# Retention slot reordered on TensorE, and the last output products and stores with it

## The chip, the cores and the metric

The kernel runs on one core of a Trainium2 chip. The metric is the device time in microseconds. Five engines work side by side and meet at semaphores: TensorE (PE, matmuls), VectorE (DVE), ScalarE (ACT), GpSimd (POOL) and SyncE (SP), which here only issues DMA transfers. An engine takes its instructions strictly in the order of the program, so an instruction that waits holds up everything behind it on its engine. Before the change the kernel took 467.58 us (median of 3 runs, 467.53 to 468.03).

## The reference

Three stages, for 2 sequences of 768 tokens and 512 channels (8 heads of 64):

```python
# 1. retention, per head
for t in range(S):
    state = gamma * state + outer(k[:, :, t], v[:, :, t])
    y[:, :, t] = scale * einsum('bhd,bhde->bhe', q[:, :, t], state)
# 2. low-rank mix over the tokens, then a channel MLP
h = xt @ U @ V                    # xt: tokens last; rank 32
u = x + h.transpose(0, 2, 1)
x = u + relu(u @ w_ch1) @ w_ch2   # 512 -> 2048 -> 512
# 3. spatial gating
h = relu(x @ w_in); u, v = halves of h
v_n = normalised v
gated = u * (w_spatial @ v_n + b_spatial)
out = gated @ w_out               # 512 -> 512
```

## The kernel before, in words

**Retention.** The work is cut into 8 items (`NI`), each a pair of heads of one batch entry; items 0 to 3 are the first sequence. An item has 6 chunks of 128 tokens (`NC`), in two groups g = 0, 1 of three (`G`). For item i TensorE runs:

- `scores(i, g)`: k times q inside a chunk, for both heads, into banks 0 and 1 (`sc_ps`). 64 rows of the array by 128 columns. VectorE (`mask_a`) and ACT (`sc_copy`) take them out, and GpSimd (`mask_b`) applies the second mask.
- `kv(i, c0, c1)`: key-value products of chunks c0 to c1, each 64x64 per head, into bank 4 and, for the fifth, into the unused end of another bank (`kv_out`). They read the keys that ACT has weighted in `decay_k(i)`, which needs the decay table `tab`. VectorE makes the five running states from them (`states`), one after the other.
- `outputs(i, g)`: for each chunk the state before it times q (line 1499), and then the masked scores times v (line 1505), into banks 2 and 3 (`y_ps`). The last chunk reads the fifth state. ACT copies them out (`xt_copy`).
- `turn(i, g)`: six transposes of the outputs, which ACT (`xn_copy`) and VectorE (`xn_rest`) split into a rounded part and its remainder.
- `down(i)`: times U, and `up(i)`: times V. `up` writes 768 columns into two banks, and VectorE adds them to the item's output (`u_add`), which makes `u`.

The token mixing of an item runs in the slot of the next: iteration i of the loop at line 1550 has the scores of i, the transposes of i-1, the products and outputs of i, and `down` and `up` of i-1. All buffers are double (`k = i % 2`). SyncE loads q and k of item i+2 when the scores of item i are done, its table and values when the outputs of item i are done.

**The rest.** The channel MLP runs in 24 steps (`product`, `ch2`), then come the input projection and the spatial product. All large products are split in a rounded part and a remainder, three matmuls for one, and seven block products replace eight (`ORDER` is the order in which the seven are taken; `S_OF` and `T_OF` name sums of weight or token blocks that ACT rounds and VectorE takes the remainder of). The last seven (`out_product`) make the output of the second sequence. Three of its four blocks are sums of two results (`sum_oc`), stored by `store_block`; the fourth is copied by ACT and stored in two halves of 192 KB.

Of the kernel before, what the change touches and what calls it, by code (L numbers as in the profile page):

```python
# [5 lines left out]
def retention_mlp_spatial_gating_kernel(  # L6
# [40 lines left out]
    with ctx:  # L47
# [263 lines left out]
        NN = NT * NP  # L311

# [100 lines left out]
        ORDER = (0, 3, 2, 1, 4, 5, 6)  # L413
        ORDER_B = (0, 3, 2, 1, 4, 5, 6)
# [5 lines left out]
        def _(sp):  # L420
# [83 lines left out]
            sp.wait_ge(stored, 16 * (CT + 1))  # L504
# [92 lines left out]
        def _(act):  # L597
# [284 lines left out]
            def last_copy(m):  # L882
                if m == 0:
                    for c in range(2, CT):
                        act.wait_ge(stage_free[c], 16)
                act.wait_ge(op_done, 7 + m)
                nc.scalar.activation(stage[:, 2 + m, 0:HS], xo_ps[m][:, 0:HS], ACT.Copy).then_inc(last_sb, 1)
# [74 lines left out]
            round_os(2)  # L962
            round_ob(4)
            round_ob(5)
            copy_op(1)
            copy_op(2)
            round_os(3)
# [6 lines left out]
        def _(dve):  # L974
            nc.vector.memset(raw(hh[0])[:, 0, :], 0.0).then_inc(idle_zeroed, 1)
            nc.vector.memset(kv_ps[:, :], 0.0).then_inc(zeroed, 1)
            nc.vector.memset(kv_out(NC - 2), 0.0).then_inc(zeroed, 1)
# [12 lines left out]
            def states(i, c0, c1):  # L990
                k = i % 2
                dve.wait_ge(kv_done, 2 * i + (2 if c0 else 1))
                for c in range(c0, c1):
                    if c:
                        dve.wait_ge(state_done, (NC - 1) * i + c)
                    if c == 0:
                        m = nc.vector.tensor_copy(st[k][:, 0, :], kv_out(0))
                    else:
                        m = nc.vector.scalar_tensor_tensor(
                            out=st[k][:, c, :], in0=st[k][:, c - 1, :], scalar=tab[k][:, 4 * P:4 * P + 1],  # L1000
                            in1=kv_out(c), op0=ALU.mult, op1=ALU.add)
# [27 lines left out]
            def u_add(i):  # L1029
                for h in range(2):  # L1030
                    dve.wait_ge(h_done, 2 * i + h + 1)
                    s = batch_of(i) * S + h * HS
                    nc.vector.tensor_tensor(u[:, pair_of(i), s:s + HS], (h_ps, p_ps)[h][:, 0:HS],
                                            xT[i % 2][:, h * HS:(h + 1) * HS], ALU.add).then_inc(u_done, 1)
# [111 lines left out]
            dve.wait_ge(zeroed, 2)  # L1146
# [4 lines left out]
            for i in range(1, NI):  # L1151
                mask_a(i, 0)
# [21 lines left out]
                u_add(i - 1)  # L1174
            xn_rest(NI - 1, 0)

            for t in range(NT):
                for j in range(NP):
# [42 lines left out]
                    if n == 1:  # L1221
                        u_add(NI - 1)
# [105 lines left out]
            def rest_os(s):  # L1328
                dve.wait_ge(os_hi, s + 1)
# [17 lines left out]
            def rest_ob(q):  # L1347
                dve.wait_ge(ob_hi, ORDER_B.index(q) + 1)
# [10 lines left out]
            def sum_oc(n):  # L1359
                ps, p, i, j = ((zo_ps, po1, 0, 0), (xo_ps, po5, 1, 1), (yo_ps, po16, 0, 1))[n]  # L1360
                dve.wait_ge(op_done, 4 + n)
                dve.wait_ge(op_copied, (1, 2, 3)[n])
                for c in range(2 * i, 2 * i + 2):
                    dve.wait_ge(stage_free[c], 16)
                for m in range(2):
                    k = nc.vector.tensor_tensor(stage[:, 2 * i + m, j * HS:(j + 1) * HS], ps[m][:, 0:HS], p[:, m, :],
                                                ALU.add)
                k.then_inc(oc_sum, 1)
# [61 lines left out]
            rest_ob(1)  # L1430
            rest_os(2)
            rest_ob(4)
            rest_ob(5)
            rest_os(3)
# [7 lines left out]
        def _(pe):  # L1442
# [21 lines left out]
            def kv(i, c0, c1):  # L1464
                k, r = i % 2, i // 2
                if c0 == 0:
# [3 lines left out]
                    else:  # L1470
                        pe.wait_ge(k_decayed, i + 1)
                        pe.wait_ge(v_loaded[k], 16 * r + 16)
                        pe.wait_ge(state_done, (NC - 1) * i)
                for c in range(c0, c1):
# [3 lines left out]
                    for a in range(2):  # L1478
                        h = slice(a * DH, (a + 1) * DH)
                        m = mm(kv_out(c)[h, h], kd[k][:, c, h], att[k][:, 3, c * P + a * DH:c * P + (a + 1) * DH],  # L1480
# [3 lines left out]
            def outputs(i, g):  # L1484
# [11 lines left out]
                for c in range(first, (g + 1) * G):  # L1496
                    for a in range(2):
# [12 lines left out]
            def turn(i, g):  # L1510
                pe.wait_ge(xt_done, 2 * i + g + 1)
                pe.wait_ge(eye_loaded, 16)
                if g and i:
                    pe.wait_ge(u_done, 2 * i - 1)
# [5 lines left out]
            def down(i):  # L1520
                pe.wait_ge(xn_lo, 2 * i + 2)
                pe.wait_ge(ust_lo, 1)
                if i == NI - 1:
                    pe.wait_ge(u_done, 2 * i)
# [4 lines left out]
            def up(i):  # L1529
                pe.wait_ge(p_lo, i + 1)  # L1530
                pe.wait_ge(v_lo, 1)
                for h in range(2):
                    mm((h_ps, p_ps)[h][:, 0:HS], pst[:, :], vst[:, h * HS:(h + 1) * HS],
# [7 lines left out]
            keep_busy(2)  # L1541
            scores(0, 0)
            keep_busy(2)
            pe.wait_ge(zeroed, 2)
# [5 lines left out]
            for i in range(1, NI):  # L1550
                scores(i, 0)
                turn(i - 1, 0)
                turn(i - 1, 1)
                if i == 1:
                    scores(i, 1)
                kv(i, 0, NC - 2)
                kv(i, NC - 2, NC - 1)
                if i > 1:
                    scores(i, 1)
                down(i - 1)  # L1560
                outputs(i, 0)
                outputs(i, 1)
                up(i - 1)
# [36 lines left out]
            def ch2(n, g):  # L1600
                h, c = g // CT, g % CT
                k, j = n % 2, n % NP
                if c == 0:
# [3 lines left out]
                    else:  # L1607
                        pe.wait_ge(w2_lo, 2 * n + h - 1)
                if j == 0 and n and h == 0:
# [49 lines left out]
            product(0, 0)  # L1659
            product(0, 1)  # L1660
# [81 lines left out]
            def out_product(q):  # L1742
                n = ORDER.index(q)
                o = (xo_ps, zo_ps, xo_ps, yo_ps, xo_ps, yo_ps, xo_ps)[q]
                if q in S_OF:
                    pe.wait_ge(os_lo, S_OF[q] + 1)
# [4 lines left out]
                pe.wait_ge(ob_lo, ORDER_B.index(q) + 1)  # L1751
# [15 lines left out]
                if q == 6:  # L1767
                    pe.wait_ge(oc_sum, 2)
                for m in range(2):
                    c = slice(m * P, (m + 1) * P)  # L1770
# [6 lines left out]
                    if m == 1 or q == 6:  # L1777
# [77 lines left out]
```

## Time and profile before

One execution was profiled. It took 468.86 us, and its span, from the first to the last instruction, is 466.9 us.

| engine | busy us | share of the span | instructions |
| --- | --- | --- | --- |
| TensorE, matmuls | 458.2 | 98% | 3128 |
| TensorE, weight loads | 409.0 | 88% | 3128 |
| VectorE | 351.3 | 75% | 772 |
| ScalarE | 253.6 | 54% | 592 |
| GpSimd | 48.1 | 10% | 52 |

The granted TensorE clock is at full speed in the whole span. The chain of work that ended last is TensorE for 94% of it. A matmul's time in the profile overlaps that of the next, so what a group of matmuls costs is read from the start of one group to the start of the next, and not from their durations. A matmul of 32-bit operands in the retention stage leaves two records. The column with 64*128 or the like is the part of the array that it uses (rows by columns).

### The profile page before, as it was taken

Reading aid. Unit: us, or ns where it says so; the run is one execution under the profiler, and the core shown is the slowest. Engines: PE = TensorE matmul, PEld = TensorE weight load, DVE = VectorE, ACT = ScalarE, POOL = GpSimd, SP = SyncE. Lnnn points to the kernel's source line nnn. Section 1 sums busy time; section 2 is a strip of 40 time slices with the busy share of each in tenths; the row PEclk is TensorE's granted clock in tenths of the full one; section 3 lists DMA queues with packets and bytes.
Section 4 is the critical chain, followed back from the end, with each engine's and each line's share of the span. In section 5 each row is a group of like instructions: output and inputs, shape, how many; then the busy total and the mean of one; then the engine's idle time right before and its main releaser. Section 6 shows DMA issues by size and latency. Waiting matters only on the chain.

```text
span 466.9 us, 8670 instructions
## 1 busy us (share of the span) xinstructions
PE 458.2 (98%) x3128; PEld 409.0 (88%) x3128; DVE 351.3 (75%) x772; ACT 253.6 (54%) x592; POOL 48.1 (10%) x52
## 2 busy tenths in 40 slices
PE   8899999999999999999999999999999999999995
PEld 4788898899999999888888999988888789999995
DVE  4788879977889978874855976765813998895783
ACT  1666756546667655843464655733523765564451
POOL 2178970000000000000100000000100001000000
PEclk9999999999999999999999999999999999999999
DMA  8989801433332343201220343302105002041003
GB/s 275 406 298 333 298 3 46 136 135 136 135 126 92 127 137 97 94 24 66 91 91 1 102 130 115 108 1 91 45 1 202 1 0 93 0 155 71 0 1 136
DMA packets 20889, 51.36 MB, mean 110 GB/s; under 512 B 1520, under 2 KB 3952, under 8 KB 19568
## 3 DMA queue, kind: packets, MB, share of 16 engines
q1 hardware_dynamic: 20432, 50.29, 31.3%
q8 instruction: 26, 0.43, 0.4%
q10 hardware_dynamic: 416, 0.53, 0.4%
q14 instruction: 15, 0.12, 0.1%
HBM read 47.66 MB, written 3.15 MB: 109 GB/s over the span
## 4 chain that ended last, share of the span: by engine, by line
PE 94%; DVE 2%; DMA 2%; ACT 1%; issue 0%; DVEq 0%
PE bank L1615 10%; PE bank L1613 10%; PE bank L1616 9%; PE bank L1594 9%; PE bank L1596 9%; PE bank L1597 8%; PE bank L1719 3%; PE bank L1721 3%; PE bank L1722 3%; PE bank L1460 3%; PE bank L1654 2%; PE bank L1653 2%; PE bank L1655 2%; PE bank L1505 2%; PE bank L1499 2%; PE bank L1737 2%
## 5 line engine op out<-in xcount | busy, mean ns | idle before, releaser
L1594 PE MATMUL bank<-bh,w1c 128*128 128x256 f32 x336 | 94.7, 282 | 0.3 <-DVE hl L1099 0.3
L1597 PE MATMUL bank<-bh,w1c 128*128 128x256 f32 x336 | 94.7, 282 | 0.0
L1596 PE MATMUL bank<-bl,w1c 128*128 128x256 f32 x336 | 94.6, 282 | 0.0
L1615 PE MATMUL bank<-hl,w2h 128*128 128x512 f32 x192 | 75.9, 395 | 0.0
L1613 PE MATMUL bank<-hh,w2h 128*128 128x512 f32 x192 | 75.8, 395 | 0.0
L1616 PE MATMUL bank<-hh,w2l 128*128 128x512 f32 x192 | 74.7, 389 | 0.0
L1594 PEld LDWEIGHTS bank<-bh,w1c 128*128 128x128 f32 x336 | 63.5, 189 | 7.0 <-issue 0.5
L1091 DVE TENSOR_TENSOR c<-bank,p 128x256 f32<-128x256 f32 x72 | 30.4, 423 | 51.1 <-PE bank L1597 29.8
L1596 PEld LDWEIGHTS bank<-bl,w1c 128*128 128x128 f32 x336 | 63.4, 189 | 5.4
L1597 PEld LDWEIGHTS bank<-bh,w1c 128*128 128x128 f32 x336 | 63.4, 189 | 0.0
L672 ACT ACTIVATE p<-bank 128x256 f32<-128x256 f32 x72 | 27.5, 381 | 45.4 <-PE bank L1597 44.3
L1616 PEld LDWEIGHTS bank<-hh,w2l 128*128 128x128 f32 x192 | 36.1, 188 | 7.9
L687 ACT ACTIVATE hh<-c 128x256 fp32r<-128x256 f32 (+1 forms) x48 | 25.1, 524 | 30.6 <-DVE c L1091 30.6
L647 ACT ACTIVATE w1c<-wsum 128x256 fp32r<-128x256 f32 x96 | 35.1, 410 | 8.4 <-DVE wsum L1050 6.3
L1615 PEld LDWEIGHTS bank<-hl,w2h 128*128 128x128 f32 x192 | 36.6, 191 | 2.2
L1613 PEld LDWEIGHTS bank<-hh,w2h 128*128 128x128 f32 x192 | 36.2, 188 | 2.5
L1063 DVE TENSOR_TENSOR w2l<-w2raw,w2h 128x512 fp32r<-128x512 f32 x46 | 31.4, 683 | 7.2 <-ACT w2h L664 7.2
L1058 DVE TENSOR_TENSOR w1c<-wsum,w1c 128x256 fp32r<-128x256 f32 x92 | 36.4, 415 | 0.0
L571 POOL TENSOR_SCALAR vare<-mv 128x4 f32<-128x4 f32 x3 | 0.7, 227 | 322.8 <-DVE mv L1124 322.8
L664 ACT ACTIVATE w2h<-w2raw 128x512 fp32r<-128x512 f32 x48 | 29.7, 620 | 0.0
L1719 PE MATMUL bank<-wsph,vh 128*128 128x384 f32 x84 | 28.1, 335 | 0.0
L1099 DVE SCALAR_TENSOR_TENSOR hl<-c,hh 128x256 fp32r<-128x256 f32 (+1 forms) x48 | 26.5, 551 | 0.8 <-ACT hh L687 0.8
(179 smaller groups left out, 948.3 us busy)
## 6 DMA issues: line engine op xcount, KB each, us to landing
w1raw<-w SPq DMA_DIRECT2D x24, 512.0 KB, 5.3
w2raw<-w SPq DMA_DIRECT2D x24, 512.0 KB, 4.1
att<-attn SPq DMA_DIRECT2D x7, 1152.0 KB, 7.8
att<-attn SPq DMA_DIRECT2D x10, 384.0 KB, 5.7
out_T<-stage SPq DMA_DIRECT2D x7, 384.0 KB, 2.5
wsp_raw<-w_sp SPq DMA_DIRECT2D x1, 2304.0 KB, 9.1
winraw<-w_in SPq DMA_DIRECT2D x4, 512.0 KB, 4.9
tab<-decay SPq DMA_DIRECT2D x7, 258.0 KB, 5.0
```

Of the source, the lines that this page charges most:

```text
L647: nc.scalar.activation(w1c[k][:, 0, q, :], w_operand(k, q), ACT.Copy).then_inc(w1_hi, 1)
L664: nc.scalar.activation(w2h[h][:, :], w2raw[n % 2][:, h, :], ACT.Copy).then_inc(w2_hi, 1)
L1058: nc.vector.tensor_tensor(w1c[k][:, 1, q, :], w_operand(k, q), raw(w1c[k])[:, 0, q, :], ALU.subtract).then_inc(w1_lo, 1)
L1063: nc.vector.tensor_tensor(w2l[h][:, :], w2raw[n % 2][:, h, :], raw(w2h[h])[:, :], ALU.subtract).then_inc(w2_lo, 1)
L1091: nc.vector.tensor_tensor(o, b, a[:, :], ALU.add).then_inc(c_sum, 1)
L1594: mm(o, w1c[k][:, 0, q, s], bh[:, q, c, :], start=(opens and c == 0), stop=False, skip_group_check=True)
L1596: mm(o, w1c[k][:, 0, q, s], bl[:, q, c, :], start=False, stop=False, skip_group_check=True)
L1597: m = mm(o, w1c[k][:, 1, q, s], bh[:, q, c, :], start=False, stop=(c == 1), skip_group_check=True)
L1613: mm(ch_ps[c][:, :], w2h[h][:, s], hh[k][:, h, :], start=(j == 0 and h == 0), stop=False, skip_group_check=True)
L1615: mm(ch_ps[c][:, :], w2h[h][:, s], hl[k][:, h, :], start=False, stop=False, skip_group_check=True)
L1616: m = mm(ch_ps[c][:, :], w2l[h][:, s], hh[k][:, h, :], start=False, stop=last, skip_group_check=True)
L1719: mm(o, vh[k][q][:, s, :], wsph[:, q, s, :], start=(q == 1 and s == 0), stop=False, skip_group_check=True)
```

## The change

In the retention stage:

- `up(i-2)` runs after `turn(i-1, 1)`, an item later than before, into banks 2 and 3 (`up_ps`), which the outputs of item i take over afterwards. Item 6's `up` runs after the first product of the MLP, item 7's stays where it was.
- the key-value products of chunks 0 to 3 of item i+1 run after `outputs(i, 1)`; that of the fifth chunk of item i runs between `outputs(i, 0)` and `outputs(i, 1)`, into the end of bank 1, once ACT has copied the scores. `outputs(i, 1)` waits for the fourth state at its start and for the fifth ahead of its last chunk.
- on ACT, `decay_k(i+1)` runs before `xt_copy(i, 0)`; on VectorE the states and the sums of `u` are spread over the item.

In the last block: q = 5 comes before q = 4, the third and fourth sums of weights are rounded in the other order (`S_ORDER`), the stores go in the order (0, 0), (0, 1), (1, 1), and block (1, 1) is summed, awaited and stored by halves.

```diff
-        def kv_out(c):
+        def kv_out(i, c):
-            return kv_ps[:, c * P:(c + 1) * P] if c < NC - 2 else y_ps[1][:, GW:GW + P]
+            return kv_ps[:, c * P:(c + 1) * P] if c < NC - 2 else (y_ps if i < 2 else sc_ps)[1][:, GW:GW + P]
...
+        def up_ps(i):
+            return y_ps if i < NI - 1 else (h_ps, p_ps)
...
-        ORDER = (0, 3, 2, 1, 4, 5, 6)
-        ORDER_B = (0, 3, 2, 1, 4, 5, 6)
+        ORDER = (0, 3, 2, 1, 5, 4, 6)
+        S_ORDER = (0, 1, 3, 2)
...
-            for n, (i, j) in enumerate(((0, 0), (1, 1), (0, 1))):
-                sp.wait_ge(oc_sum, n + 1)
-                store_block(i, j)
-            for m in range(2):
-                sp.wait_ge(last_sb, m + 1)
-                sp.dma_start(out[2 + m, :, S:S + HS], stage[:, 2 + m, 0:HS]).then_inc(stored, 16)
+            for j in range(2):
+                sp.wait_ge(oc_sum, j + 1)
+                store_block(0, j)
+            for j in (1, 0):
+                for m in range(2):
+                    if j:
+                        sp.wait_ge(oc_sum, 3 + m)
+                    else:
+                        sp.wait_ge(last_sb, m + 1)
+                    sp.dma_start(out[2 + m, :, S + j * HS:S + (j + 1) * HS], stage[:, 2 + m, j * HS:(j + 1) * HS]
+                                 ).then_inc(stored, 16)
...
-                xt_copy(i, 0)
                 if i < NI - 1:
                     decay_k(i + 1)
+                xt_copy(i, 0)
                 xt_copy(i, 1)
...
# VectorE, the loop over the items
+                if i > 1:
+                    states(i, 0, G)
                 mask_a(i, 0)
...
-                states(i, 0, NC - 2)
-                states(i, NC - 2, NC - 1)
-                if i > 1:
+                    states(i, 0, NC - 2)
+                    states(i, NC - 2, NC - 1)
+                else:
+                    u_add(i - 2, 0)
+                    states(i, G, NC - 2)
+                    u_add(i - 2, 1)
                     mask_a(i, 1)
+                    states(i, NC - 2, NC - 1)
                 p_rest(i - 1)
...
-                u_add(i - 1)
...
# TensorE
+                if i > 1 and c1 == NC - 1:
+                    pe.wait_ge(sc_copied, 2 * i + 2)
...
-                pe.wait_ge(state_done, (NC - 1) * i + (G - 1 if g == 0 else NC - 1))
+                pe.wait_ge(state_done, (NC - 1) * i + (G - 1 if g == 0 else NC - 2 if i > 1 else NC - 1))
...
+                if i > 1:
+                    pe.wait_ge(u_done, 2 * (i - 2) + g + 1)
...
+                    if c == NC - 1:
+                        pe.wait_ge(state_done, (NC - 1) * (i + 1))
...
                 turn(i - 1, 0)
                 turn(i - 1, 1)
+                if i > 1:
+                    up(i - 2)
+                scores(i, 1)
                 if i == 1:
-                    scores(i, 1)
-                kv(i, 0, NC - 2)
-                kv(i, NC - 2, NC - 1)
-                if i > 1:
-                    scores(i, 1)
+                    kv(i, 0, NC - 2)
+                    kv(i, NC - 2, NC - 1)
                 down(i - 1)
                 outputs(i, 0)
+                if i > 1:
+                    kv(i, NC - 2, NC - 1)
                 outputs(i, 1)
-                up(i - 1)
+                if i < NI - 1:
+                    kv(i + 1, 0, NC - 2)
...
             turn(NI - 1, 0)
             product(0, 0)
+            up(NI - 2)
             product(0, 1)
...
# the last products
-                if q == 6:
-                    pe.wait_ge(oc_sum, 2)
                 for m in range(2):
+                    if q == 6:
+                        pe.wait_ge(oc_sum, 3 + m)
...
-                    if m == 1 or q == 6:
+                    if m == 1 or q == 6 or q == 4:
                         i.then_inc(op_done, 1)
```

TensorE, item 7 of the retention stage. Before, from its first scores to the first transposes of the item itself (1460 scores, 1516 transposes, 1480 key-value products, 1526 `down`, 1499 and 1505 outputs, 1533 `up`):

```order
L1460 MATMUL bank<-att_55 128x128 x6
L1516 MATMUL bank<-ident,xT_53 128x128 x6
L1480 MATMUL bank<-att_55,kd_56 64x64 x10
L1460 MATMUL bank<-att_55 128x128 x6
L1526 MATMUL bank<-xn,ust 128x256 x6
L1499 MATMUL bank<-qd_57,st_58 64x128 x4
L1505 MATMUL bank<-am_54,att_55 64x128 x6
L1499 MATMUL bank<-qd_57,st_58 64x128 x6
L1505 MATMUL bank<-am_60,att_55 64x128 x6
L1533 MATMUL bank<-vst,pst 128x384 x2
L1516 MATMUL bank<-ident,xT_59 128x128 x3
```

The same place now; the line numbers moved (1479 scores, 1539 transposes, 1556 `up`, 1547 `down`, 1524 and 1530 outputs, 1501 key-value products), and the first row is the last of item 6's slot:

```order
L1501 MATMUL bank<-att_55,kd_56 64x64 x8
L1479 MATMUL bank<-att_55 128x128 x6
L1539 MATMUL bank<-ident,xT_53 128x128 x6
L1556 MATMUL bank<-vst,pst 128x384 x2
L1479 MATMUL bank<-att_55 128x128 x6
L1547 MATMUL bank<-xn,ust 128x256 x6
L1524 MATMUL bank<-qd_57,st_58 64x128 x4
L1530 MATMUL bank<-am_54,att_55 64x128 x6
L1501 MATMUL bank<-att_55,kd_56 64x64 x2
L1524 MATMUL bank<-qd_57,st_58 64x128 x6
L1530 MATMUL bank<-am_60,att_55 64x128 x6
L1539 MATMUL bank<-ident,xT_59 128x128 x3
```

Eight of the ten key-value products moved behind the outputs of the item ahead, two between the outputs, and `up` behind the transposes.

VectorE at an item of the same stage, before (986 masks, 1018 remainder of `xn`, 997 and 999 states, 1025 and 1027 the remainder of `down`'s result, 1013 weighted q, 1033 sum of `u`):

```order
L986 TENSOR_TENSOR am_54<-bank,tab_99 128x384
L1018 TENSOR_TENSOR xn<-bank,xn 128x3x128 x2
L997 COPY st_52<-bank 128x128
L999 SCALAR_TENSOR_TENSOR st_52<-st_52,tab_99,bank 128x128 x4
L986 TENSOR_TENSOR am_60<-bank,tab_99 128x384
L1025 TENSOR_TENSOR prest<-bank,pst 32x128
L1027 TENSOR_TENSOR pst<-bank,prest 32x128
L1013 TENSOR_TENSOR qd_57<-att_55,tab_100 128x640
L1033 TENSOR_TENSOR u<-bank,xT_59 128x384 x2
```

And now (1006 and 1008 states, 995 masks, 1027 remainder of `xn`, 1041 sum of `u`, 1034 and 1036 the remainder of `down`'s result, 1022 weighted q):

```order
L1006 COPY st_58<-bank 128x128
L1008 SCALAR_TENSOR_TENSOR st_58<-st_58,tab_100,bank 128x128 x2
L995 TENSOR_TENSOR am_54<-bank,tab_100 128x384
L1027 TENSOR_TENSOR xn<-bank,xn 128x3x128 x2
L1041 TENSOR_TENSOR u<-bank,xT_59 128x384
L1008 SCALAR_TENSOR_TENSOR st_58<-st_58,tab_100,bank 128x128
L1041 TENSOR_TENSOR u<-bank,xT_59 128x384
L995 TENSOR_TENSOR am_60<-bank,tab_100 128x384
L1008 SCALAR_TENSOR_TENSOR st_58<-st_58,tab_100,bank 128x128
L1034 TENSOR_TENSOR prest<-bank,pst 32x128
L1036 TENSOR_TENSOR pst<-bank,prest 32x128
L1022 TENSOR_TENSOR qd_51<-att_49,tab_99 128x640
```

Three states moved to the front of the item, the fifth to behind the second mask, and the two sums, now of the item two back, in between.

## Rows read from the trace of the kernel before

**Rows 1.** Busy time by engine in item 7 of the retention stage

```profile
core 0: us, PE busy (x) PEld busy (x) DVE busy (x) ACT busy (x) POOL busy (x), PEclk, DMA share, GB/s
58.27:65.45 7.18, 7.18 (x103) 6.36 (x103) 5.17 (x13) 3.93 (x10) 7.18 (x7) 1.00 0.01 3
```

**Rows 2.** TensorE in order of time, one item; start, duration, line, tile, count

```profile
43.72 0.94 PE L1460 MATMUL bank<-att 64*128 64x128 f32 x12
44.59 0.87 PE L1516 MATMUL bank<-ident,xT 128*128 128x128 f32 x6
45.40 0.80 PE L1480 MATMUL bank<-att,kd 128*64 128x64 f32 x20
46.13 0.94 PE L1460 MATMUL bank<-att 64*128 64x128 f32 x12
47.00 0.97 PE L1526 MATMUL bank<-xn,ust 128*128 128x256 f32 x6
...
49.03 0.82 PE L1499 MATMUL bank<-qd,st 128*64 128x128 f32 x12
49.69 0.83 PE L1505 MATMUL bank<-am,att 128*64 128x128 f32 x12
50.45 0.61 PE L1533 MATMUL bank<-vst,pst 128*128 128x384 f32 x2
50.98 0.94 PE L1460 MATMUL bank<-att 64*128 64x128 f32 x12
```

**Rows 3.** TensorE in order of time, transposes among MLP products

```profile
67.21 0.49 PE L1516 MATMUL bank<-ident,xT 128*128 128x128 f32 x3
67.45 0.36 PE L1594 MATMUL bank<-bh,w1c 128*128 128x256 f32 x1
```

**Rows 4.** ACT and VectorE in the same item, and the duration of a state

```profile
44.71 0.49 ACT L606 ACTIVATE am<-bank 128x384 f32<-128x384 f32 x1 [0.93 <-PE bank L1460]
...
45.70 1.02 DVE L1018 TENSOR_TENSOR xn<-bank,xn 128x384 fp32r<-128x384 f32 x2 [0.38 <-ACT xn L628]
...
L999 DVE SCALAR_TENSOR_TENSOR st<-st,tab,bank x32: 346/347/349, 10.0 to 62.7; 128x128 f32<-128x128 f32 x32
```

**Rows 5.** VectorE and TensorE in order of time, a matmul released by VectorE

```profile
72.65 0.42 DVE L1099 SCALAR_TENSOR_TENSOR hl<-bank,hh 128x256 fp32r<-128x256 f32 x1 [0.16 <-ACT hh L687]
...
73.22 0.36 PE L1594 MATMUL bank<-bh,w1c 128*128 128x256 f32 x1 [0.30 <-DVE hl L1099]
```

**Rows 6.** The end of item 1 in order of time: table load, weighted keys, next scores

```profile
13.22 0.33 SPq L431 DMA_DIRECT2D tab<-decay  x1
...
20.80 1.01 ACT L616 ACTIVATE kd<-att,tab 128x320 f32<-128x320 f32 x2 [0.38 <-DMA tab<-decay]
...
21.89 0.94 PE L1460 MATMUL bank<-att 64*128 64x128 f32 x12
```

**Rows 7.** Loads of the decay tables, line 431

```profile
DMA to landing us min/median/max: 4.0/5.0/7.6
```

**Rows 8.** Loads of the values, line 427

```profile
DMA to landing us min/median/max: 4.6/5.7/8.2
```

**Rows 9.** Stores of 384 KB in the last block, line 493

```profile
DMA to landing us min/median/max: 2.5/2.5/2.5
```

**Rows 10.** The two last stores, line 501, issued at 461.8 and 462.7

```profile
L501 SPq DMA_DIRECT2D out_T<-stage x2: 344/344/345, 461.8 to 462.7; - x2
...
DMA to landing us min/median/max: 2.7/3.2/3.7
```

**Rows 11.** Waits of SyncE at the end: total, times, longest

```profile
SPq L504 <- DMA out_T<-stage: 3.2, 1, 3.2
```

**Rows 12.** DMA from 463.3 to 467, busy tenths in 40 slices, and its instruction queue

```profile
DMA  9999899994000000001010100000000000000000
...
q8 instruction: 1, 0.02, 1.6%
```

More of the change, by code:

```diff
@@ L961, in _ @@
             copy_op(0)
-            round_os(2)
-            round_ob(4)
+            round_os(3)
             round_ob(5)
             copy_op(1)
+            round_ob(4)
+            round_os(2)
             copy_op(2)
-            round_os(3)
             round_ob(6)
@@ L976, in _ @@
             nc.vector.memset(kv_ps[:, :], 0.0).then_inc(zeroed, 1)
-            nc.vector.memset(kv_out(NC - 2), 0.0).then_inc(zeroed, 1)
+            nc.vector.memset(kv_out(0, NC - 2), 0.0).then_inc(zeroed, 1)
+            nc.vector.memset(kv_out(2, NC - 2), 0.0).then_inc(zeroed, 1)
             def mask_a(i, g):
@@ L991, in states @@
                 k = i % 2
-                dve.wait_ge(kv_done, 2 * i + (2 if c0 else 1))
+                dve.wait_ge(kv_done, 2 * i + (2 if c1 == NC - 1 else 1))
                 for c in range(c0, c1):
@@ L996, in states @@
                     if c == 0:
-                        m = nc.vector.tensor_copy(st[k][:, 0, :], kv_out(0))
+                        m = nc.vector.tensor_copy(st[k][:, 0, :], kv_out(i, 0))
                     else:
@@ L1027, in p_rest, with u_add @@
                 nc.vector.tensor_tensor(pst[r, :], p_ps[r, P:2 * P], prest[r, :], ALU.add).then_inc(p_lo, 1)
[L1029 to L1034, printed above, removed]
+            def u_add(i, h):
+                dve.wait_ge(h_done, 2 * i + h + 1)
+                s = batch_of(i) * S + h * HS
+                nc.vector.tensor_tensor(u[:, pair_of(i), s:s + HS], up_ps(i)[h][:, 0:HS],
+                                        xT[i % 2][:, h * HS:(h + 1) * HS], ALU.add).then_inc(u_done, 1)
             def weight_sums(n, ss):
@@ L1145, in _ @@
             decay_q(0)
-            dve.wait_ge(zeroed, 2)
+            dve.wait_ge(zeroed, 3)
             states(0, 0, NC - 2)
@@ L1173, in _ @@
                     decay_q(i + 1)
-                u_add(i - 1)
             xn_rest(NI - 1, 0)
+            u_add(NI - 2, 0)
+            u_add(NI - 2, 1)
             for t in range(NT):
@@ L1221, in _ @@
                     if n == 1:
-                        u_add(NI - 1)
+                        u_add(NI - 1, 0)
+                        u_add(NI - 1, 1)
                     if final:
@@ L1347, in rest_ob @@
             def rest_ob(q):
-                dve.wait_ge(ob_hi, ORDER_B.index(q) + 1)
+                dve.wait_ge(ob_hi, ORDER.index(q) + 1)
                 if q in T_OF:
@@ L1359, in sum_oc @@
             def sum_oc(n):
-                ps, p, i, j = ((zo_ps, po1, 0, 0), (xo_ps, po5, 1, 1), (yo_ps, po16, 0, 1))[n]
+                ps, p, i, j = ((zo_ps, po1, 0, 0), (yo_ps, po16, 0, 1), (xo_ps, po5, 1, 1))[n]
                 dve.wait_ge(op_done, 4 + n)
-                dve.wait_ge(op_copied, (1, 2, 3)[n])
+                dve.wait_ge(op_copied, (1, 3, 2)[n])
                 for c in range(2 * i, 2 * i + 2):
@@ L1365, in sum_oc @@
                 for m in range(2):
+                    if n == 2 and m:
+                        dve.wait_ge(op_done, 7)
                     k = nc.vector.tensor_tensor(stage[:, 2 * i + m, j * HS:(j + 1) * HS], ps[m][:, 0:HS], p[:, m, :],
                                                 ALU.add)
-                k.then_inc(oc_sum, 1)
+                    if n == 2 or m:
+                        k.then_inc(oc_sum, 1)
             sums_v(0, range(0, 2))
@@ L1430, in _ @@
             rest_ob(1)
+            rest_os(3)
+            rest_ob(5)
+            rest_ob(4)
             rest_os(2)
-            rest_ob(4)
-            rest_ob(5)
-            rest_os(3)
             sum_oc(0)
@@ L1512, in turn @@
                 pe.wait_ge(eye_loaded, 16)
-                if g and i:
-                    pe.wait_ge(u_done, 2 * i - 1)
                 for c in range(G):
@@ L1532, in up @@
                 for h in range(2):
-                    mm((h_ps, p_ps)[h][:, 0:HS], pst[:, :], vst[:, h * HS:(h + 1) * HS],
+                    if i < NI - 1:
+                        pe.wait_ge(xt_done, 2 * i + 3 + h)
+                    mm(up_ps(i)[h][:, 0:HS], pst[:, :], vst[:, h * HS:(h + 1) * HS],
                        start=True, stop=True).then_inc(h_done, 1)
@@ L1541, in _ @@
             keep_busy(2)
+            pe.wait_ge(zeroed, 3)
             scores(0, 0)
             keep_busy(2)
-            pe.wait_ge(zeroed, 2)
             kv(0, 0, NC - 2)
@@ L1608, in ch2 @@
                         pe.wait_ge(w2_lo, 2 * n + h - 1)
+                if n == 0 and h == 0 and c < 2:
+                    pe.wait_ge(u_done, 2 * NI - 3 + c)
                 if j == 0 and n and h == 0:
@@ L1750, in out_product @@
                     wh, wl = w_out_block(wouth, i, j), w_out_block(woutl, i, j)
-                pe.wait_ge(ob_lo, ORDER_B.index(q) + 1)
+                pe.wait_ge(ob_lo, ORDER.index(q) + 1)
                 if q in T_OF:
```

15 lines of the change are left out of this document (7 added, 8 removed).

## The prediction, made before the result was known

> **What bounds the kernel now.** I read the page's busy shares first, then a window and the instructions of the retention stage in order of time, then the stores at the end. The page has TensorE busy for 458.2 of 466.9 us at the full granted clock; in item 7 of the retention stage it is busy for all 7.18 us, with VectorE at 5.17 and GpSimd at 7.18 beside it [rows 1]. So the span is TensorE's own row of work, with the start before it and the last store behind it, and a change counts only where it shortens that row, puts a stall into it, or moves the last store. This one touches the eight retention items (11 to 65 us) and the last 20 us. The rest keeps its order but for two matmuls.
>
> In that stage item follows item every 7.26 to 7.29 us; the reader should take the period from 43.72 to 50.98 [rows 2] and look at the tile sizes. Scores use the array as 64*128; transposes, `down` and `up` as 128*128; key-value products and outputs as 128*64. A change of form costs time. Twelve records of 128 columns take 0.66 us among outputs (49.03 to 49.69), where the form stays. The twelve of a score group fill 0.87 (43.72 to 44.59), 0.21 more. The six transposes fill 0.81, where six at the same pace of 0.11 take 0.66: 0.15 more. A period has seven such changes (scores, transposes, key-value, scores, `down`, outputs, `up`, scores); at the mean of 0.18 they are 1.26 us of it. Where the form stays nothing is lost: three transposes among products of the same form take 0.24 [rows 3].
>
> **The change part by part.**
>
> *Retention, what goes.* In items 2 to 7 `up` now stands behind the transposes, both 128*128, and the key-value products stand behind outputs, both 128*64. Seven changes of form become five: 2 x 0.18 = 0.36 us less per item, with the same matmuls. That alone would make the period 6.92. The Trainium skill names the cause (TensorEngine Tiling (Array Packing), section Key Properties: switching the tiling mode, not merely the tile, drains TensorE). Rows 2 agree with it at 0.18 us a switch; taken alone it makes the kernel some 2 us faster, which is part of the first rival.
>
> *Retention, the wait of `down`.* Key-value products (0.73) no longer stand between the transposes and `down`; `up` does, for 0.35 (its 0.53 of rows 2 less a switch). Counted from the item's first score matmul: scores to 0.87; transposes and `up` take 0.66 + 0.05 + 0.35 + 0.10 (two halves of the switches around them), to 2.03; scores to 2.90. But `down` needs the second remainder of `xn`, and that chain hangs on the first scores and not on TensorE's order behind them: ACT copies the scores at 44.71, 0.99 after the start, then makes two copies of `xn`, and VectorE's second remainder ends at 45.70 + 1.02 = 46.72, which is 3.00 after the start [rows 4]. TensorE starts 0.15 after the end of what it waits for (72.65 + 0.42 = 73.07, start at 73.22) [rows 5]. So `down` starts at 3.15 instead of 2.90, a stall of 0.25. Before it started at 3.28 (47.00), with 0.13 to spare.
>
> *Retention, the wait of the last state.* The product of chunk 5 now stands between outputs(i, 0) and outputs(i, 1), and the last chunk of outputs(i, 1) reads the state made from it. `down` and outputs(i, 0) take 2.03 (47.00 to 49.03), so the product starts at 5.18. It has two pairs of records at 0.06 (0.73 less 0.15 for ten pairs), the last ends some 0.22 after its start (45.40 + 0.80 is 0.07 beyond the next group's start), so it ends at 5.46; VectorE starts 0.05 later (as ACT does: 43.72 + 0.94 = 44.66, then 44.71), a state takes 0.35 [rows 4], and TensorE follows 0.15 later, at 6.01. To fill that it has the product's 0.12 and two chunks of outputs, 0.44: until 5.74. A stall of 0.27. VectorE is free by then: the two remainders end at 3.00, and two sums (0.47 each), a state and a mask end near 4.9. Queued behind the wait are the rest of the outputs, the next key-value products and the next scores, all of TensorE's row, so nothing absorbs it.
>
> Then come 0.22 + 0.66 of outputs, 0.47 of key-value products (eight pairs) and 0.10 for the switch: the next item starts at 7.46. Against 7.28 that is 0.18 slower; 0.52 of stalls for 0.36 of switches. Items 2 to 6: 5 x 0.18 = 0.9 us.
>
> *Retention, item 1.* Its end now holds the first products of item 2, and they need `decay_k(2)`. That waits for the decay table, issued at 13.22; ACT starts at 20.80 and ends at 21.81 [rows 6]. So the products start at 21.96 and item 2's scores at 21.96 + 0.47 + 0.10 = 22.53 instead of 21.89: 0.64 later. Before, that wait lay beside the `up` of item 0. The table took 7.6 us to land, at the shortest 4.0 [rows 7]; in the best case the loss goes, so 0 to 0.7.
>
> *Retention, item 7 and the rest.* No next item and one switch less: 7.00 against 7.18, 0.18 less. The `up` of item 6 moves among the first products and costs its 0.35 there. ACT has roundings ahead of the score copy in items 6 and 7: 0.1 together. The values of the next item must have landed 0.5 us before its start and no longer in its middle: issued at its predecessor's start, they took 5.7 us in the middle case and 8.2 at most [rows 8], against 6.9 at which they are wanted. I take nothing, with 0 and 1.3 as ends. GpSimd's masks are wanted no earlier: nothing.
>
> Sum of the stage: 0.64 + 0.9 - 0.18 + 0.35 + 0.1 = 1.8 us.
>
> *The last block.* The seven products keep their matmuls and their form. In the new order each should find its operands: the fifth (q = 5) takes the third rounding of weights, made in the place of what was the third before; the last (q = 6) waits for a sum on each half, 0.55 us of VectorE inside the half's 1.04 of TensorE. I take 0, and 0.4 if VectorE comes late. What changes is the queue of stores. A store of 384 KB landed 2.5 us after its issue [rows 9]. The two of 192 KB at the end, issued at 461.8 and 462.7, were right behind one of 384 KB and took 2.7 and 3.7 us [rows 10], and SyncE waited 3.2 for the last [rows 11]. Its last packets went out alone, long after the others, in a window that also holds a block of 16 KB of instructions [rows 12]. Now half of that 384 KB goes out 1 us, half 2 us before the last two. Bounds: nothing, if the block still cuts in, and 1.8 us, if the last store lands in 1.9 (2.5 less 0.6 for half the bytes). Whether the block cuts in without the profiler too I can't see. I take the middle, 0.9.
>
> The Trainium skill (Runtime: NRT & Kernel Launch, section Instruction fetch mechanics) has an engine fetch its program in blocks of 16 KiB through a DMA queue of its own, and rows 12 agree. TensorE's program is a dozen waits longer now, so by that rule the block may come earlier and still cut in; the sum would then be 1.8 and not 0.9.
>
> **Sum.** 466.9 + 1.8 - 0.9 = 467.8 us of span. The profiled execution took 468.86, which is 1.28 above the median; I put the difference onto the median: 467.58 + 0.9 = 468.5 us.
>
> **The rivals.**
> 1. *The switches win.* If one of the two stalls is not there, a period is 7.20 and the stage ends 1.8 - 6 x 0.26 = 0.2 later; with neither, 1.3 earlier. With 0.9 to 1.8 from the store the kernel takes 464.5 to 466.9 us. For it: the switches are plain in rows 2. Against it: each link of both chains has a row, and neither chain depends on TensorE's new order. It decides from the point where both answers come back within what TensorE has in hand, 2.90 and 0.56 us.
> 2. *The store gives all back.* 1.8 - 1.8: 467.6 us, no change. For it: the lonely packets; against it: the longer program.
> 3. *Nothing from the store, and loads late.* The tail is the profiler's own, and the values of an item or two land after 6.9: 467.58 + 1.8 + 0.4 to 1.3 = 469.8 to 470.7. For it: DMA carries loads through most of the stage; against it: the middle case has 1.2 to spare.
> 4. *The forms are not brought together.* If key-value products among outputs cost a switch after all (64 columns against 128), an item has three more: 6 x 3 x 0.18 = 3.2 us, 471.7. Against it: both are listed as 128*64 [rows 2].
>
> **How the numbers follow.** Forecast, both stalls and part of the store: 0.50, at 468.5, its own range 467.8 to 469.5. Rival 1: 0.16. Rival 2: 0.19. Rival 3: 0.11. Rival 4: 0.04. A measurement of this kernel can tell about 0.2% (0.94 us) from no change, so below 466.6 is faster and above 468.5 slower: the forecast stands on that edge. Slower: 0.27 of the forecast, 0.15 of rivals 3 and 4, 0.03 of rival 2 = 0.45. Faster: 0.14 of rival 1 and 0.01 of rival 2. The same: the remaining 0.40. The range, 466.6 to 469.8, leaves out the better part of rival 1 and most of 3 and 4.
>
> **What would show it.** In the changed profile: a period of 7.4 to 7.5 us; `down` 3.15 after the item's first scores, released by VectorE's remainder of `xn`; near 0.27 of idle before the last chunk of outputs(i, 1), released by a state; the products of item 2 right behind `decay_k(2)`; item 7's transposes 1.4 us after 65.45; no stall in the last seven products; and the last store landing less than 3 us after its issue. A period under 7.25 makes the forecast wrong, and so does a stall in the last products or a wait for values.

## The result, and the profile after

The changed kernel takes 468.45 us (median of 12 runs, 467.96 to 469.31), the kernel before 467.56 in the same measurement: a ratio of 1.0023, with a 95% interval of 1.0014 to 1.0032. That is 0.9 us slower, a small change, but the interval is clear of no change. The forecast was 468.5. Its steps were less good than its sum, as the experiments show.

The profiled execution took 468.00 us with a span of 466.0; before it was 468.86 with a span of 466.9. So in the two profiled executions the changed kernel is 0.9 us *shorter*, and over all runs 0.9 us longer. Two things pull apart: TensorE's row of work got longer, and in the profiled execution the last store landed sooner.

One item after the change, TensorE in order of time (start, duration, line, tile; the lines are those named in the section on the change, and 1524 and 1530 are the outputs). It answers to [rows 2].

```profile
44.39 0.94 PE L1479 MATMUL bank<-att 64*128 64x128 f32 x12
45.26 0.88 PE L1539 MATMUL bank<-ident,xT 128*128 128x128 f32 x6
45.89 0.60 PE L1556 MATMUL bank<-vst,pst 128*128 128x384 f32 x2
46.41 0.94 PE L1479 MATMUL bank<-att 64*128 64x128 f32 x12
47.44 0.97 PE L1547 MATMUL bank<-xn,ust 128*128 128x256 f32 x6
48.34 0.66 PE L1524 MATMUL bank<-qd,st 128*64 128x128 f32 x8
48.83 0.82 PE L1530 MATMUL bank<-am,att 128*64 128x128 f32 x12
49.48 0.28 PE L1501 MATMUL bank<-att,kd 128*64 128x64 f32 x4
49.60 1.06 PE L1524 MATMUL bank<-qd,st 128*64 128x128 f32 x12
50.49 0.82 PE L1530 MATMUL bank<-am,att 128*64 128x128 f32 x12
51.14 0.64 PE L1501 MATMUL bank<-att,kd 128*64 128x64 f32 x16
51.71 0.94 PE L1479 MATMUL bank<-att 64*128 64x128 f32 x12
```

The period is 7.32 us where it was 7.28. Two stalls are in it. The second scores take 1.03 to the start of `down` (46.41 to 47.44), and 0.87 where nothing is waited for: 0.16. And the group of line 1524 at 49.60 takes 0.89 where twelve such records take 0.66: 0.23. VectorE in the same item has both releasers, the second remainder of `xn` and the fifth state:

```profile
46.37 1.02 DVE L1027 TENSOR_TENSOR xn<-bank,xn 128x384 fp32r<-128x384 f32 x2 [0.34 <-ACT xn L636]
...
49.82 0.35 DVE L1008 SCALAR_TENSOR_TENSOR st<-st,tab,bank 128x128 f32<-128x128 f32 x1 [0.78 <-PE bank L1501]
```

The remainder ends at 47.39 and `down` starts at 47.44; the state ends at 50.17 and TensorE goes on at 50.22. Each handover took 0.05 us.

Items 6 and 7 have a third wait that items 2 to 5 lack. The second scores of item 7 start 2.27 after its first ones, where item 5 has 2.02 (46.41 less 44.39). They wait for VectorE's first mask (995), which now stands behind the weighted q (1022) and three states:

```profile
58.20 1.53 DVE L1022 TENSOR_TENSOR qd<-att,tab 128x640 f32<-128x640 f32 x1
...
60.73 0.55 DVE L995 TENSOR_TENSOR am<-bank,tab 128x384 f32<-128x384 f32 x1
...
61.33 0.94 PE L1479 MATMUL bank<-att 64*128 64x128 f32 x12 [0.18 <-DVE am L995]
```

The mask ends at 61.28, 0.05 before the scores. The weighted q took 1.53 us here and 0.88 two items earlier (at 43.52); why it took longer is not shown. Before the change this mask stood ahead of the states and ended 0.80 before the same scores (59.87, and 60.67). In item 6 the same wait is 0.13.

The end of item 1 in order of time, which answers to [rows 6]: SyncE's table load, ACT's weighted keys, the products of item 2, its scores.

```profile
13.50 0.33 SPq L434 DMA_DIRECT2D tab<-decay  x1
...
20.73 1.02 ACT L624 ACTIVATE kd<-att,tab 128x320 f32<-128x320 f32 x2 [0.63 <-DMA tab<-decay]
...
21.80 0.69 PE L1501 MATMUL bank<-att,kd 128*64 128x64 f32 x16 [0.17 <-ACT kd L624]
22.41 0.94 PE L1479 MATMUL bank<-att 64*128 64x128 f32 x12
```

The way into the MLP: item 7's first transposes start at 66.07 (before: 65.45), and item 6's `up` stands among the products for 0.36.

```profile
66.07 0.55 PE L1539 MATMUL bank<-ident,xT 128*128 128x128 f32 x3
...
67.17 0.52 PE L1556 MATMUL bank<-vst,pst 128*128 128x384 f32 x2
67.53 0.28 PE L1620 MATMUL bank<-bh,w1c 128*128 128x256 f32 x1
```

The last stores of 192 KB and SyncE's last wait, beside [rows 10, 11]:

```profile
L508 SPq DMA_DIRECT2D out_T<-stage x4: 332/338/444, 460.6 to 463.6; - x4
...
DMA to landing us min/median/max: 1.8/1.9/2.4
```

```profile
SPq L512 <- DMA out_T<-stage: 1.4, 1, 1.4
```

The last wait is 1.4 us instead of 3.2. TensorE's last matmul starts at 462.75, before at 461.82.

### The profile page after: what moved, and what is told of

Its sections match the earlier page's. It is cut to its first block, busy times and chain, and to the rows that moved or that the text cites. A ratio compares the mean times of both kernels' runs of the same rounds, so it can differ in the third digit from the quotient of the medians.

```text
span 466.0 us, 8685 instructions
## 1 busy us (share of the span) xinstructions
PE 459.2 (99%) x3128; PEld 409.6 (88%) x3128; DVE 350.8 (75%) x773; ACT 253.9 (54%) x592; POOL 48.2 (10%) x52
## 4 chain that ended last, share of the span: by engine, by line
PE 91%; DVE 4%; ACT 2%; DMA 2%; issue 1%; DVEq 0%
PE bank L1643 10%; PE bank L1641 10%; PE bank L1644 9%; PE bank L1620 9%; PE bank L1622 9%; PE bank L1623 9%; PE bank L1751 3%; PE bank L1750 3%; PE bank L1748 3%; PE bank L1682 2%; PE bank L1681 2%; PE bank L1683 2%; PE bank L1766 2%; PE bank L1524 2%; PE bank L1479 2%; PE bank L1530 2%
```

## Experiments

Each ran beside the kernel before on the same chip. Ratios are to it, with 95% intervals.

### The last block alone, and the retention change alone

`tail_only` is the kernel before with the diff of the last block (`ORDER`, `S_ORDER`, the stores, `sum_oc`); `ret_only` has all the rest of the diff and not that. The measurements of this section were taken on three chips at different times, so kernels of different groups are compared by their ratios.

> The kernel before with only the last block changed (order of the last products, sums and stores by halves). Theory A, the late packets of the last store belong to the profiled execution: the last product's row ends where it did, so the time is that of before within 0.2 us. Theory B, my recorded sum: the new order of stores brings 0.9 us, and the retention stage costs 1.8: 466.7 us, ratio 0.998. In the trace both expect the last store of 192 KB to land 1.9 us after its issue.

> The kernel before with only the retention change. Theory A: the whole difference, +0.9 us, 468.5. Theory B: 1.8 us slower, 469.4. In the trace a period of 7.32 us as in the changed kernel, and the first matmul of the last block 0.9 later than before.

| kernel | median us | ratio | last matmul at |
| --- | --- | --- | --- |
| before | 467.43 | | 461.82 |
| `tail_only` | 467.57 | 1.0005 [0.9991, 1.0020] | 462.18 |
| `ret_only` | 468.50 | 1.0025 [1.0011, 1.0039] | 462.71 |

The slowdown is the retention stage's, and the last block alone gives nothing that can be measured; the interval ends short of the 0.9 us that I had booked (0.9991 is 0.4 us). In `ret_only` the period is 7.33 and the last block starts 0.89 later (448.33 against 447.44), as expected. Of the two theories A holds for both medians. One number went against both: in `tail_only` the last store is not landed 1.9 after its issue. SyncE waited 2.1 for it:

```profile
SPq L509 <- DMA out_T<-stage: 2.1, 1, 2.1
```

The first line of its item 1 tells what to take off when two traces are compared:

```profile
13.42 0.94 PE L1468 MATMUL bank<-att 64*128 64x128 f32 x12
```

Up to there `tail_only` has the code of before, which was at 13.11. So executions differ by 0.3 us in their first 13, and the 0.27 by which the changed kernel is late there (13.38) need not be an effect of the change; below it is not counted as one.

### The fifth product put ahead, then the wait of `down` split

`fifth_early` moves one call on TensorE:

```diff
+                if i > 1:
+                    kv(i, NC - 2, NC - 1)
                 outputs(i, 0)
-                if i > 1:
-                    kv(i, NC - 2, NC - 1)
                 outputs(i, 1)
```

`fifth_split` has this and, in `down`, a split wait; `split_only` is the changed kernel with the split wait alone:

```diff
-                pe.wait_ge(xn_lo, 2 * i + 2)
+                pe.wait_ge(xn_lo, 2 * i + 1)
                 pe.wait_ge(ust_lo, 1)
                 for c in range(NC):
+                    if c == G:
+                        pe.wait_ge(xn_lo, 2 * i + 2)
```

> The changed kernel with the fifth chunk's product of items 2 to 7 ahead of outputs(i, 0) instead of behind it, no other edit. If the stall for the last state is a stall of its own (0.18 plus 0.05 for restarting), each item gets 0.23 shorter: period 7.09, six times 0.23 = 1.4 us, 467.1 us. If another wait, hidden behind it, takes its place (VectorE's masks and sums, which are in the same queue), the period stays at 7.25 or more and the kernel within 0.4 us of the changed one.

> fifth_early, and down waits for the second remainder of xn only ahead of its fourth matmul, for the first remainder ahead of its first. The stall of 0.16 ahead of down goes too: period 6.93, which is the switches' gain alone (7.28 less 2 x 0.18), and the kernel takes 467.1 - 6 x 0.16 = 466.1 us. Rival: the time comes back elsewhere, since VectorE's and ACT's chains from one item's scores to its outputs are then the longest thing in the item: period 7.05 or more, 466.8 us or more.

> The changed kernel with the wait of down split (first remainder ahead of its first matmul, second ahead of its fourth), and the fifth product left where it is. If the two stalls are independent, down starts 0.16 earlier in each item and the state stall stays at 0.18 to 0.23: period 7.16, 467.5 us. If the product's earlier start is eaten by VectorE's queue ahead of the last state (its second mask), the state stall grows and the period stays above 7.25.

| kernel | state stall | `down` stall | period of item 5 | median us | ratio |
| --- | --- | --- | --- | --- | --- |
| after (from the result) | 0.23 | 0.16 | 7.32 | 468.45 | 1.0023 [1.0014, 1.0032] |
| `split_only` | 0.23 | 0 | 7.17 | 467.64 | 1.0009 [1.0000, 1.0017] |
| `fifth_early` | 0 | 0.16 | 7.09 | 466.72 | 0.9985 [0.9971, 0.9999] |
| `fifth_split` | 0 | 0 | 6.93 | 466.17 | 0.9976 [0.9963, 0.9990] |

`fifth_split`, TensorE in order of time, the same item (1549 is `down`):

```profile
43.12 0.94 PE L1479 MATMUL bank<-att 64*128 64x128 f32 x12
...
45.15 0.94 PE L1479 MATMUL bank<-att 64*128 64x128 f32 x12
46.02 0.98 PE L1549 MATMUL bank<-xn,ust 128*128 128x256 f32 x6
46.92 0.34 PE L1501 MATMUL bank<-att,kd 128*64 128x64 f32 x4
47.09 0.61 PE L1524 MATMUL bank<-qd,st 128*64 128x128 f32 x8
47.53 0.83 PE L1530 MATMUL bank<-am,att 128*64 128x128 f32 x12
48.18 0.83 PE L1524 MATMUL bank<-qd,st 128*64 128x128 f32 x12
48.84 0.83 PE L1530 MATMUL bank<-am,att 128*64 128x128 f32 x12
```

`down` starts 0.87 after the scores (46.02 less 45.15), and the second group of 1524 takes 0.66 (48.18 to 48.84). The last three periods were expected at 7.16, 7.09 and 6.93. In items 2 to 5 the stalls add up and nothing takes their place.

In items 6 and 7 something does. With the split wait alone, item 6 takes 7.44 us (the changed kernel 7.35) and item 7 still 7.01, because the second scores wait for the mask. `fifth_early` has item 7 down to 6.64; in `fifth_split` it is back at 7.01, because its outputs now wait for GpSimd's mask:

```profile
53.53 0.94 PE L1479 MATMUL bank<-att 64*128 64x128 f32 x12 [0.20 <-DVE am L995]
```

```profile
61.97 0.88 PE L1530 MATMUL bank<-am,att 128*64 128x128 f32 x12 [0.32 <-POOL am L529]
```

(The first line is item 6 of `split_only`, the second item 7 of `fifth_split`.) So the second step, from `fifth_early` to `fifth_split`, is 0.55 us at the median and not the 6 x 0.16 = 0.96 that I had expected; the two intervals overlap.

Back to item 5. With the product ahead of outputs(i, 0) it starts 1.7 us before the last chunk wants the state (46.92, and 48.18 + 0.44); in the changed kernel it started 0.56 before (49.48, and 49.60 + 0.44). And 6.93 against 7.28 leaves 0.35 for two changes of form fewer, with the same matmuls: 0.175 each.

The Trainium skill (TensorEngine Tiling (Array Packing), section Key Properties) has the switch of tiling mode drain TensorE; the traces agree that a switch costs time, 0.175 us each here.

### Where item 1's time goes

In the kernels above that have item 2's products at the end of item 1, that item took 8.97 to 9.78 us, where it took 8.78 before. `tab3` gives the decay table a third buffer, so that item 2's is loaded at the start and the later ones an item earlier; `k2_back` takes the four products back into item 2, puts `decay_k(2)` behind both copies of item 1's outputs, and VectorE's first three states of item 2 behind its two remainders.

```diff
# tab3, on fifth_split
-        tab = [None, None]
+        tab = [None, None, at("tab2", C_AT, [P, DEC])[0]]
...
+            load_tab(2, 2)
...
# k2_back, on fifth_split: TensorE
+                if i == 2:
+                    kv(i, 0, NC - 2)
                 scores(i, 1)
...
-                if i < NI - 1:
+                if 1 < i < NI - 1:
                     kv(i + 1, 0, NC - 2)
```

> fifth_split with a third buffer for the decay table, so that item 2's table is loaded at the start, ahead of its q and k, and no longer after item 0. In four traces the products of item 2 waited for decay_k(2), which waited for that table, and item 1 took 8.97 to 9.77 us. If that wait is a loss of its own, item 1 takes 8.6 to 8.7 us here (8.54 from its first scores to the end of its outputs' row in fifth_split was 7.89; plus 0.57 of products and 0.15 of the form change), and the kernel 0.5 us less than fifth_split in the middle case (0.3 to 1.1): 465.7 us. If values or q and k of item 2 are what comes late next, nothing is gained: 466.2.

> fifth_split with the first four products of item 2 back in item 2, behind the transposes and up, and decay_k(2) behind both copies of item 1's outputs. One change of form more (0.18), no wait for the table. Theory: item 1 plus item 2 take 0.18 more than in tab3, so about 15.8 us against 16.1 in fifth_split, and the kernel 465.9 us. Rival, the wait costs nothing off the profile: 466.3 us.

`tab3` took 466.76 us (ratio 0.9991 [0.9981, 1.0002]), no better than `fifth_split`, and in its trace item 1 took 9.68 us instead of the 8.6 to 8.7 expected, so my theory fell and the rival stood. `decay_k(2)` no longer waits, and TensorE still does:

```profile
19.72 1.01 ACT L626 ACTIVATE kd<-att,tab 128x320 f32<-128x320 f32 x2
...
21.95 0.69 PE L1503 MATMUL bank<-att,kd 128*64 128x64 f32 x16 [0.87 <-issue]
```

"issue" means that the profile shows no releaser. The values of item 2, issued at 13.36 in that execution, landed 8.5 us later:

```profile
L430 SPq DMA_DIRECT2D att<-attn x1: 433/433/433, 13.4 to 13.4; - x1
...
DMA to landing us min/median/max: 8.5/8.5/8.5
```

13.36 + 8.5 = 21.9, and the products start at 21.95. In the trace of the changed kernel the two are as close: the values, issued at 13.87, landed after 7.8 us, at 21.7, and `decay_k(2)` ended at 21.75. So the products of item 2 wait for table *and* values. Both stand in transfers that fill the DMA engines: the DMA share of item 1 is 1.04 in `tab3`, and in `tail_only` 1.03, at 407 GB/s (below). That loading one of them earlier puts the other one later fits `tab3`'s 8.5 us against 8.0 in `fifth_split`, but one trace of each doesn't show it.

```profile
13.42:22.18 8.76, 7.63 (x105) 6.25 (x104) 6.89 (x15) 6.42 (x14) 2.02 (x2) 1.00 1.03 407
```

`k2_back` took 465.97 us (0.9972 [0.9961, 0.9982]). Its items 1 and 2 together take 15.36 us (13.30 to 28.66) where `fifth_split` has 16.11, 0.75 less, and more than the 0.3 that I had expected: item 1 ends without a wait for transfers, after 7.45. It varies from execution to execution (7.18 to 8.17 in the three kernels with this order), so its share of a median can't be read from one trace. At the median `k2_back` is 0.8 us below `tab3`, measured beside it, but its ratio is within the interval of `fifth_split` (0.9976), so whether item 1's wait was worth anything against that kernel stays open.

### The last store again, and the fastest version

`best` is `tab3` with GpSimd's fourth remainder of tokens behind item 7's masks, `k2_best` is `k2_back` with the same edit. Both were run with the new last block and with the old one (`_oldtail`).

```diff
                 elif i == 6:
-                    first_token_rest(range(0, 4))
-            first_token_rest(range(4, NQ))
+                    first_token_rest(range(0, 3))
+            first_token_rest(range(3, NQ))
```

> tab3, and GpSimd takes three instead of four of the first remainders of tokens ahead of the masks of item 7. In fifth_split the first outputs of item 7 stood 0.32 for that mask. Theory: 0.3 us less than tab3, 465.4 us. Rival: the fourth remainder then comes late for the first products of the MLP, and nothing is gained.

> best with the last block and its stores as in the kernel before. Theory A (the late packets of the last store belong to the profiled execution): the same time as best within 0.3 us. Theory B (the new order of stores brings 0.9 us): 0.9 us more than best.

> k2_back, and GpSimd takes three instead of four of the first remainders of tokens ahead of the masks of item 7. If what is left of item 7's wait (0.3 us) is a loss of its own, 465.7 us and a row of TensorE that ends 0.3 earlier than in k2_back (last matmul at 459.8 instead of 460.1); if the fourth remainder then comes late, 466.0.

> k2_best with the last block and its stores as in the kernel before; the third pair for this question, after before against tail_only (0.1 slower with the new order) and best_oldtail against best (0.5 faster with it). If the new order is worth nothing where no profiler is, the medians differ by less than 0.3 us; if it is worth 0.9, by 0.6 or more. The profiled execution should show the last store landing 1 us later than in k2_best in either case.

| last block | median old | median new | new less old | last wait old | last wait new |
| --- | --- | --- | --- | --- | --- |
| before, `tail_only` | 467.43 | 467.57 | +0.14 | 3.2 | 2.1 |
| `ret_only`, after | 468.50 | 468.45 | -0.05 | 2.5 | 1.4 |
| `best_oldtail`, `best` | 466.92 | 466.43 | -0.49 | 2.6 | 1.4 |
| `k2_best_oldtail`, `k2_best` | 466.00 | 465.45 | -0.55 | 1.5 | 1.4 |

(`ret_only` and after were measured at different times, the others side by side.) In the profiled executions the new order shortens the last wait in all four pairs, by 0.1 to 1.2 us. In the medians it is worth about 0.25 on average, between nothing and 0.55, and in each pair the intervals of the two ratios overlap. My two limits, under 0.3 and over 0.6, left the last two pairs in between. `tail_only` by itself allows 0.4 us at most; the last two pairs by themselves allow 0.9 too. What the new order is worth in the mean execution, nothing or some tenths, stays open. For `k2_best_oldtail` I had expected the last store 1 us later than in `k2_best`, and the waits are 1.5 and 1.4: a miss.

In the four profiled executions with the old order, time and last wait go together: they lie 1.28, 0.66 and 0.35 above their medians with waits of 3.2, 2.5 and 2.6, and 1.22 below with 1.5. So the tail seems to differ from execution to execution; that the profiler makes it longer, as theory A has it, isn't shown.

The long waits go with the block of instructions of [rows 12]. From 454 us on, each of the four traces with the old order has one on queue q8, as here in `ret_only`:

```profile
q8 instruction: 1, 0.02, 0.8%
```

Of the nine traces with the new order two have one, `tail_only` and `tab3`, with last waits of 2.1 and 2.0 us; the seven without have 1.4. It isn't shown that the block holds up the packets (`k2_best_oldtail` has one and waits 1.5), only that no wait over 1.5 came without it.

`k2_best` is the fastest kernel of the study: 465.45 us (5 runs, 464.39 to 465.51), ratio to before 0.9955 [0.9941, 0.9968]. The edit on GpSimd did what it should: item 7 takes 6.45 us instead of 7.01, and from its first scores to the first matmul of the last block `k2_best` takes 388.7 us (57.08 to 445.80), `k2_back` 389.3 (56.48 to 445.73). Its last matmul is at 460.21 and not at the 459.8 that I had expected, since item 1 took 0.7 longer in this execution (8.17 against 7.45). `best` has 0.3 us less than `tab3` at the median, as expected, though the two intervals overlap.

## Why the prediction was right, and where it was not

The total was met by luck: two errors of like size cancelled. The stage was booked at +1.8 us and the store at -0.9; the runs give about +1.0 (`ret_only`, 0.5 to 1.8) and between nothing and 0.55.

- *Seven changes of form become five.* Right: 0.36 booked, 0.35 shown by `fifth_split`.
- *The wait of `down`.* Right in its place and its releaser, too large: 0.25 booked, 0.16 measured. The remainder ended at 3.00 as I had it. TensorE followed 0.05 later and not 0.15.
- *The wait of the last state.* Right in place and releaser: 0.27 booked, 0.23 measured (0.18 of idle and 0.05 to get going again, for which I had no term). The product started at 5.09 instead of 5.18, and again TensorE followed after 0.05, so that it went on at 5.83 and not at 6.01.
- *The period.* This is the term that was mis-sized: 7.46 booked, 7.32 measured, so +0.04 an item and not +0.18. 0.20 of the difference is the handover, taken twice at the 0.15 of [rows 5] and measured twice at 0.05; 0.05 the other way is getting going again. [Rows 5] is a wait of another stage; I had no row of this one, and took it as a value and not as a bound. "A period under 7.25 makes the forecast wrong" was not met, by 0.07.
- *Item 1.* Its `decay_k(2)` and the products right behind it are as forecast, 0.64 booked. In the trace of the changed kernel it is 0.25 (9.03 less 8.78), in the other four 0.2 to 1.0. Of the 0.39 too much, 0.10 is the handover; the rest is that item 1 started 0.27 later while the table, issued at 13.50, landed when it had before, 7.2 us after its issue instead of 7.6. I named the table; `tab3` shows that the values are as late.
- *Item 7 and `up(6)`.* 0.18 less and 0.35 more booked, 0.17 and 0.36 measured, but the first agreement is luck. Item 7's two stalls measured 0.06 and 0.23 where 0.52 was booked, and its second scores waited 0.25 for VectorE's first mask, a wait for which the prediction has no term: the change puts three states ahead of that mask, and I had followed only VectorE's work behind it. For ACT's roundings 0.1 was booked, and they decide nothing (ACT's score copy in item 7 ends at 60.62, the mask at 61.28). As a whole the stage is shorter than booked: item 7's transposes start 0.62 after 65.45, 0.27 of which is the start of the execution, not the 1.4 that I gave.
- *The last block.* Right: from its first matmul to its last 14.42 us, before 14.38.
- *The store.* Right in the trace, and more: the last landed 1.9 after its issue and the last wait fell by 1.8. Wrong for the kernel: the profiled execution of before lay 1.28 above its median, that of the changed kernel 0.45 below. I had put the difference of spans onto the median, and that carries over a loss which the median run seems not to have: of the 35 runs of before beside `tail_only`, 7 took 468.6 us or more. That these 7 are the ones with late packets is argued, not shown.

In the trace the parts make 0.25 + 0.27 (items 2 to 6, 36.65 against 36.38) - 0.17 + 0.36 = 0.7 us. The last block starts 0.89 later (448.33), or 0.62 without the start. The medians say 0.9 to 1.1. The 0.3 between them lies within their intervals, and item 1's scatter would cover it; that is argued, not shown.

Of the rivals, the first was the nearest to deciding the sign: it needed one of the two stalls to be gone. They were there, and `fifth_early` and `fifth_split` show what the change is worth without them, 466.7 and 466.2 us. The second and third named the two answers for the store, and the truth is nearer the third (little or nothing from the store) with a stage half as dear and no values that landed late in items 3 to 7. The fourth is out: products among outputs cost no change of form, 0.12 for two pairs (49.48 to 49.60).

The Trainium skill (Runtime: NRT & Kernel Launch, section Instruction fetch mechanics) has programs come in through a DMA queue in blocks of 16 KiB. The traces agree on the block (0.02 MB on q8). That a longer program still lets it cut in, for which I had given 1.8 us, did not come true in the changed kernel's trace.

## What to carry to other kernels

Bringing instructions of one array form together paid 0.175 us a change here, but each chain of answers (VectorE, ACT, GpSimd, a load) must be checked against its new place, in every item and not in one alone: a product that feeds the last link of a chain goes as early as its bank allows, and a wait goes in front of the matmul that needs it, not in front of the group. A gain at the very end of a profiled execution is worth its size only if the other runs pay for the same loss: compare the profiled execution's own time with the median before booking it.

## What was not expected of the hardware

- A matmul followed the end of VectorE's result by 0.05 us (`down`, outputs), where another stage had shown 0.15 [rows 5].
- After a wait inside a run of equal matmuls the next pair took 0.05 us longer than the 0.11 of its neighbours, besides the idle time: the group of line 1524 at 49.60 is 0.23 longer, for 0.18 of idle.
- Executions of the same code differ by 0.3 us in their first 13 us (13.11 and 13.42), and by 0.8 in item 1 alone while transfers are queued (8.97 to 9.78, in kernels whose item 1 is the same).
